# Attention, Fourier mixing and routed experts on one core: GpSimd's folds wait for VectorE, and the order of work of the sequence transform is changed

## The chip, the cores and the metric

One core of a Trainium2 chip runs the whole program in one launch. The metric is device time in microseconds; of several runs the median counts. TensorE (PE) multiplies, VectorE (DVE), ScalarE (ACT) and GpSimd (POOL) work on elements, SyncE (SP) issues most of the DMAs. Each engine works through its own list of instructions in order; semaphores (`wait_ge`, `then_inc`) tie the lists together.

## The reference

```python
scores = scale * q @ k.T; scores += slopes * -|i - j|; mask: 0 <= i - j < 128
x = softmax(scores) @ v                       # 4 x 8 heads, 576 tokens, 64 wide
...
X = fft over tokens, then over the 512 features; mixed = real(X)
u = x + mixed; un = (u - mean) / sqrt(var + 1e-6)
x = u + relu(un @ w_ch1) @ w_ch2              # 512 -> 2048 -> 512
...
e = argmax(x @ w_gate), or the last token's expert where the local gate says so
out = softmax(gate)[e] * relu(x @ w1[e]) @ w2[e]   # 8 experts, 512 -> 1024 -> 512
```

## The kernel before

Every float32 product is made of three float16 products: an operand is split into a high half, a rounded copy (names ending in `_hi`, on ScalarE), and a low half, the rest (`_lo`, on VectorE or GpSimd).

**Attention.** The 32 heads are worked on as 16 pairs (`PAIRS`), four pairs to a batch (`PPB`). Iteration p has on TensorE the scores of pair p + 1, the transposed scores of pair p, and the sums over keys of pair p - 1 (`pv`). ScalarE has the high halves of q and k of pair p + 2 (`qk_hi_of`, L1150), the exponentials (L1159, L1160), v, `x_hi_of` (L1179) and the copy of the row of maxima (`copy_row`, L1164). VectorE has `normalise(p - 2)` (L1440 to L1448), the maxima `max_of` (L1402 to L1409), `qk_lo_of(p + 2)` (L1426), `p_lo_of` (L1433) and `neg_of` (L1419, L1421). GpSimd has, in this order, `v_lo_of(p)` (L1859, after `neg_of(p)`), `x_lo_of(p - 5)` (L1867), `fold_x(p - 3)` (L1887, L1888, and a copy of an end column, L1894, for one pair in four), `fold_d(p - 4)` (L1904) and sometimes `xl_lo_of` (L1875). The folds add and subtract mirrored tokens and features of x, so that the transform needs half of the rows. SP asks, in each iteration, for v of pair p + 2 (after `v_lo_of`), four shifts of x and its store (after `normalise`), and last for q and k of pair p + 3 (L525, after `qk_lo_of(p + 2)`).

**The transform along the sequence.** For each batch b, `spectrum(b)` (L838) makes two chunks on TensorE, numbered k = 2b + c, in banks 0 and 1 or 2 and 3 of PSUM by turns; chunk k waits until `spectrum_lo` of chunk k - 2 has read its banks (`ulo_done`). `spectrum_hi` (L1226, L1229) and `spectrum_lo` (L1508, L1510) split it. `middle_rows` makes the rows of the middle feature, for batch 0 and then for the other three; `middle_hi_of` and `middle_lo_of` split them. Once batch 0 is through, `tile_spectrum(0, 4)` (L868 to L875) transforms the first tile of tokens along the features; `copy_b` and `fold` (VectorE) and `u_q` (GpSimd, L1981, after a gather of rows of x from memory, L1955) make u of it, `moments` (L1561, L1565), `std_of` (ScalarE, L1254) and `normalise_u` (L1569, L1572) normalise it, and `transpose_un` (L884) turns it for the channel MLP. `edge()` (L957, L961) makes the last sums for the rows at a batch's edge, after a small transpose of the gate's weights (L987).

**The channel MLP.** `mlp(t)` works through 9 tiles of 2 x 128 tokens (`hidden` L908, `project` L925). Its weights arrive in 32 chunks of 512 columns, staged in a ring of 10 buffers; `w_hi_of(n)` (L1218) and `w_lo_of(n)` (L1454) split chunk n, and SP's `load_w(n)` (L530) waits for the split of chunk n - 10. `mlp(0, first=True)` waits for the chunks as it comes to them: 4 ahead of `hidden(0, 0)`, 8 ahead of `hidden(0, 2)`, 10 ahead of `project(0, 0)`, 16 ahead of `hidden(0, 4)`. Behind it come the other tiles, the routing and the experts, none of which the diff touches.

The order on each engine is written out by hand; nothing plans it.

Of the kernel before, what the change touches and what calls it, by code (L numbers as in the profile page):

```python
# [32 lines left out]
B, NH, S, DH = 4, 8, 576, 64  # L33
# [7 lines left out]
PAIRS = HEADS // 2  # L41
# [76 lines left out]
def fused_kernel(nc, qk, v, mlp_w, exp_w, w_gate, bias, seq_dft, dim_dft, ident, ident_b,  # L118
# [9 lines left out]
    with ctx:  # L128
# [381 lines left out]
        def settle(engine):  # L510


            engine.sem_inc(passed, 1)
# [148 lines left out]
        def _(pe):  # L662
# [304 lines left out]
            pe.wait_ge(table_made, 3)  # L967
            pe.wait_ge(table_clear, 2)
            spectrum(0, (0,))
            for a in range(2):  # L970
                pv(PAIRS - 1, a)
            pe.wait_ge(p_lo[0], PAIRS)
            spectrum(0, (1,))
            pe.wait_ge(x_done, PAIRS)
            pe.wait_ge(xl_split, 1)
            middle_rows(1)
            spectrum(1)
            pe.wait_ge(ulo_done, DH2)
            pe.wait_ge(middle_split, 1)
            tile_spectrum(0, 4)  # L980
# [2 lines left out]
            middle_rows(B)  # L983
            spectrum(3)
            transpose_un(0, 4, un_first)
            pe.wait_ge(ulo_done, DH2 * B)
            nc.tensor.transpose(psum[0:DC * (E + 1), 0, 0:P], wg_in.rearrange("p c e -> p (c e)"), ident_sb[:, :])\  # L987
                .then_inc(gateT_ready, 1)
            pe.wait_ge(middle_split, 2)
            edge()  # L990
            mlp(0, first=True)
# [145 lines left out]
        def _(act):  # L1137
# [74 lines left out]
            def w_hi_of(n):  # L1212
                act.wait_ge(w_loaded[n % WRING], 16 * (n // WRING + 1))
                at = W_ORDER[n]
                if at >= W_FREE and n == min(W_ORDER.index(i) for i in range(W_FREE, WCH)):
                    act.wait_ge(x_split, PAIRS)
                    act.wait_ge(xl_split, B)
                nc.scalar.activation(wparts[:, 0, at * CH:(at + 1) * CH], w_staging[n % WRING], ACT.Copy, scale=WS)\  # L1218
                    .then_inc(w_hi, 1)
# [20 lines left out]
                    nc.scalar.activation(mid_last[0:rows, 0, b:b + 1], psum[0:rows, 6, QUART:TH], ACT.Copy, scale=own)\  # L1240
                        .then_inc(middle_hi, 1)

            for n in range(W_SPEC):
                w_hi_of(n)

            def copy_b(t, first=False, at=0):
                act.wait_ge(ab_ready, t + 1)
                if not first:
# [48 lines left out]
                hidden_hi(t, 7, first)  # L1297

            spectrum_hi(0, (0,))
            x_hi_of(PAIRS - 4)  # L1300
            spectrum_hi(0, (1,))
            x_hi_of(PAIRS - 3)
            middle_hi_of(1)
            spectrum_hi(1, (0,))
            xl_hi_of(B - 1)
            x_hi_of(PAIRS - 2)
            spectrum_hi(1, (1,))
            act.wait_ge(m_clear, 1)
            x_hi_of(PAIRS - 1)
            copy_b(0, first=True, at=4)  # L1310
            w_hi_of(4)
            spectrum_hi(2, (0,))
            w_hi_of(5)
            spectrum_hi(2, (1,))
            w_hi_of(6)
            std_of(0)
            spectrum_hi(3, (0,))
            middle_hi_of(2)
            spectrum_hi(3, (1,))
            w_hi_of(7)  # L1320
            unT_hi_of(0, at=4)
            w_hi_of(8)
            mlp(0, first=True)
            mlp(1, second=True)
# [59 lines left out]
        def _(dve):  # L1384
# [97 lines left out]
            for p in range(PAIRS):  # L1482
                more = p + 1 < PAIRS
                if p > 1:
                    normalise(p - 2)
                if more:
                    max_of(p + 1, 0)
                if p + 2 < PAIRS:
                    qk_lo_of(p + 2)
                if more:  # L1490
                    max_of(p + 1, 1)
                p_lo_of(p, 0)
                if more:
                    max_of(p + 1, 2)
                    neg_of(p + 1)
                p_lo_of(p, 1)
            normalise(PAIRS - 2)
            normalise(PAIRS - 1)

            def spectrum_lo(b, chunks=range(DH2)):  # L1500

# [9 lines left out]
                                            psum[:, bank:bank + 2, 0:320].rearrange("p r (q g) -> p r q g", q=2)[:, :, :, 0:QUART],  # L1511
                                            part[0], ALU.subtract).then_inc(ulo_done, 1)

            def middle_lo_of(n):

                rows = 1 if n == 1 else B
                dve.wait_ge(middle_hi, 1 if n == 1 else B)
                for b in range(1) if n == 1 else range(1, B):
                    own = 1.0 if n == 1 else ident_sb[0:rows, b:b + 1]
                    part = [middle[0:rows, h, b * HALF:(b + 1) * HALF].rearrange("p (g r) -> p r g", r=2) for h in range(2)]  # L1520
                    nc.vector.scalar_tensor_tensor(out=part[1], in0=psum[0:rows, 6:8, 0:QUART], scalar=own, in1=part[0],
                                                   op0=ALU.mult, op1=ALU.subtract)
                    last = nc.vector.scalar_tensor_tensor(out=mid_last[0:rows, 1, b:b + 1], in0=psum[0:rows, 6, QUART:TH],
                                                          scalar=own, in1=mid_last[0:rows, 0, b:b + 1], op0=ALU.mult,
                                                          op1=ALU.subtract)
                last.then_inc(middle_split, 1)

            spectrum_lo(0)
            w_lo_of(0)
            w_lo_of(1)  # L1530
            dve.wait_ge(middle_clear, 1)
            middle_lo_of(1)

            def u_of(t, q):
                return u_sb[:, bass.ds(t % 2, 1), q, :].rearrange("p o d -> p (o d)")
# [18 lines left out]
                nc.vector.tensor_tensor(u[:, FC:D], summ[:, FC - 2:0:-1], xg[:, 0, FC:D], ALU.add)\  # L1554
                    .then_inc(up_done, 1)

            def moments(t):
                for q in range(2):
                    dve.wait_ge((up_done, uq_done)[q], t + 1)
                    settle(dve)  # L1560
                    nc.vector.bn_stats(bstat[:, q, :], u_of(t, q)).then_inc(stat_done, 1)  # L1561
                for q in range(2):
                    dve.wait_ge(stat_done, 2 * t + 1 + q)
                    settle(dve)
                    nc.vector.bn_aggr(mv[:, q, :], bstat[:, q, :]).then_inc(mv_done, 1)  # L1565
# [93 lines left out]
                if not last:  # L1659
                    x2_of(t, first)  # L1660

            dve.wait_ge(table_loaded, 1)
            nc.vector.memset(eps_sb[:, :], XS * XS * LN_EPS)
            spectrum_lo(1, (0,))

            def end_fold_d(n):

# [4 lines left out]
                                        ALU.add if n % 2 == 0 else ALU.subtract).then_inc(d_done, 1)  # L1672

            end_fold_d(PAIRS - 2)
            dve.wait_ge(eo_done, PAIRS)
            for par in range(2):
                dve.wait_ge(x_stored[par], 16 * PAIRS // 2)
            nc.vector.memset(bcopy[:, 0:1], 0.0)
            nc.vector.memset(bcopy[:, FC - 1:FC], 0.0).then_inc(m_clear, 1)
            w_lo_of(2)  # L1680
            spectrum_lo(1, (1,))
            end_fold_d(PAIRS - 1)
            fold(0, first=True, at=4)
            w_lo_of(3)
            spectrum_lo(2, (0,))
            w_lo_of(4)
            spectrum_lo(2, (1,))
            moments(0)
            w_lo_of(5)
            normalise_u(0, un_first)  # L1690
            spectrum_lo(3, (0,))
            middle_lo_of(2)
            spectrum_lo(3, (1,))
            unT_lo_of(0, at=4)
            for n in range(6, 9):
                w_lo_of(n)
            dve.wait_ge(gateT_ready, 1)
# [158 lines left out]
        def _(pool):  # L1856
# [71 lines left out]
            for p in range(PAIRS):  # L1928
                if p > 0:
                    pool.wait_ge(neg_ready, p + 1)  # L1930
                    for a in range(2):
                        v_lo_of(p, a)
                if p > 4:
                    x_lo_of(p - 5)
                if p > 2:
                    fold_x(p - 3)
                if p > 3:
                    fold_d(p - 4)
                if p % PPB == 3 and p > PPB:
                    xl_lo_of(p // PPB - 1)  # L1940
                if p in (1, 2):
                    table_part(p - 1)
# [215 lines left out]
```

## Time and profile before

| | us |
|---|---|
| median of 3 runs | 897.63 |
| lowest, highest | 895.72, 898.65 |
| profiled execution, its own time | 901.19 |
| its span, first to last instruction | 899.4 |
| mean granted clock of TensorE | 0.978 |

The times in the rows below are microseconds from the start of the span. "[1.24 <-DVE m_mem L1448]" behind a row means that the engine had been idle so long and what ended the idle time. In the granted clock, 1.00 is full speed.

### The profile page before, as it was taken

How to read it: one execution, taken by the hardware profiler on the slowest of the kernel's cores; microseconds unless marked ns; L12 is line 12 of the kernel's file. 1: busy time of each engine (PE TensorE's matmuls, PEld its weight loads, DVE VectorE, ACT ScalarE, POOL GpSimd, SP SyncE). 2: the span in 40 equal slices, each digit the busy share in tenths (PEclk: the TensorE clock that was granted, in tenths of full speed). 3: DMA queues.
4: the chain of work that ended last, by engine and by line, in shares of the span. 5: the costliest groups of instructions: out<-in, count | busy, mean ns of one | idle time of the engine just before them, and what ended most of it. 6: DMA issues, size and time to landing. Idle time of an engine off the chain costs nothing.

```text
span 899.4 us, 22524 instructions
## 1 busy us (share of the span) xinstructions
PE 847.5 (94%) x8820; PEld 610.3 (68%) x8821; DVE 549.4 (61%) x1123; ACT 307.2 (34%) x461; POOL 273.4 (30%) x289
## 2 busy tenths in 40 slices
PE   8989988989999999999999999929999999999995
PEld 4767767867666676767676767517777777777773
DVE  6899986887656575747484839768995883000000
ACT  5788887553111111111111111103333333333331
POOL 2457776602010101010111100013444444334431
PEclk9999999999999999999999999959999999999998
DMA  9455552654310101010101003405774772111100
GB/s 289 131 170 149 178 146 62 197 201 133 117 47 23 47 23 47 23 47 23 47 23 47 25 24 130 129 27 165 253 236 147 228 231 80 47 45 51 49 24 1
DMA packets 60474, 91.28 MB, mean 101 GB/s; under 512 B 7304, under 2 KB 30971, under 8 KB 60421
## 3 DMA queue, kind: packets, MB, share of 16 engines
q1 hardware_dynamic: 55061, 74.80, 27.0%
q0 software_dynamic: 5360, 15.74, 5.5%
q8 instruction: 37, 0.61, 0.3%
q14 instruction: 16, 0.13, 0.0%
HBM read 73.16 MB, written 16.57 MB: 100 GB/s over the span
## 4 chain that ended last, share of the span: by engine, by line
PE 80%; DVE 9%; DMA 3%; issue 2%; ACT 2%; SPq 2%; POOL 1%; DVEq 0%; POOLq 0%; ACTq 0%
PE psum L908 21%; PE psum L925 21%; PE psum L1085 14%; PE psum L1101 14%; DMA m_mem<-in_qk 2%; PE psum L675 2%; DVE m_mem L1405 1%; DVE arena L1426 1%; DVE arena L1433 1%; PE psum L1052 1%; PE psum L884 1%; PE psum L788 1%; PE psum L875 1%; PE psum L868 1%; PE psum L1034 1%
## 5 line engine op out<-in xcount | busy, mean ns | idle before, releaser
L908 PE MATMUL psum<-m_mem,arena 128*128 (+1 forms) x1728 | 198.5, 273 | 0.0
L925 PE MATMUL psum<-arena,m_mem 128*128 128x512 f16 x864 | 195.3, 379 | 0.0
L908 PEld LDWEIGHTS psum<-m_mem,arena 128*128 128x128 f16 x1728 | 169.5, 98 | 28.3 <-issue 0.4
L925 PEld LDWEIGHTS psum<-arena,m_mem 128*128 128x128 f16 x864 | 84.5, 98 | 90.4
L1085 PEld LDWEIGHTS psum<-m_mem,arena 128*128 x2400 | 137.1, 97 | 6.9 <-issue 1.5
L1085 PE MATMUL psum<-m_mem,arena 128*128 128x128 f16 x2400 | 139.4, 218 | 1.2 <-issue 0.6
L1101 PE MATMUL psum<-arena,m_mem 128*128 x600 | 133.4, 379 | 0.0
L1268 ACT ACTIVATE m_mem<-psum 128x512 f16<-128x512 f32 x72 | 43.0, 597 | 243.2 <-PE psum L908 243.2
L1615 DVE SCALAR_TENSOR_TENSOR m_mem<-m_mem,arena 128x512 f16<-128x512 f32 x144 | 102.8, 768 | 0.0
L1101 PEld LDWEIGHTS psum<-arena,m_mem 128*128 128x128 f16 x600 | 57.7, 98 | 65.1
L1987 POOL TENSOR_TENSOR arena<-m_mem,arena 128x1024 f16<-128x1024 f32 x9 | 19.2, 2135 | 256.5 <-ACT arena L1279 211.6
L1586 DVE SCALAR_TENSOR_TENSOR m_mem<-psum,m_mem 128x512 f16<-128x512 f32 x72 | 49.4, 687 | 50.3 <-ACT m_mem L1268 49.6
L675 PE MATMUL psum<-arena 64*128 64x256 f16 (+3 forms) x960 | 55.3, 253 | 15.7 <-DVE m_mem L1405 13.4
L2026 POOL TENSOR_TENSOR m_mem<-m_mem 128x1024 f32 (+1 forms) x25 | 51.2, 2046 | 51.8 <-ACT m_mem L1353 51.7
L1350 ACT ACTIVATE m_mem<-psum 128x1024 f32 (+1 forms) x25 | 25.6, 1024 | 113.1 <-PE psum L1085 113.1
L1633 DVE SCALAR_TENSOR_TENSOR arena<-dimdft_sb,arena 128x512 f16<-128x512 f32 x74 | 59.8, 808 | 2.5
L675 PEld LDWEIGHTS psum<-arena 64*128 64x128 f16 x960 | 37.8, 95 | 26.9 <-DVE m_mem L1405 16.1
L1597 DVE SCALAR_TENSOR_TENSOR m_mem<-psum,m_mem 128x512 f32<-128x512 f32 x18 | 11.6, 686 | 57.3 <-PE psum L925 57.3
L1859 POOL TENSOR_TENSOR m_mem<-arena,m_mem 128x320 f16<-128x320 f32 x32 | 25.2, 810 | 63.9 <-DVE m_mem L1421 46.3
L1631 DVE TENSOR_SCALAR arena<-dimdft_sb 128x512 f16<-128x512 f32 x74 | 35.4, 478 | 13.4 <-PE psum L1101 13.4
L1633 DVE SCALAR_TENSOR_TENSOR arena<-wstage,arena 128x512 f16<-128x512 f32 (+1 forms) x54 | 40.7, 754 | 3.5
L1362 ACT ACTIVATE m_mem<-psum,m_mem 128x512 f32<-128x512 f32 x25 | 17.2, 689 | 71.8 <-PE psum L1101 68.2
(242 smaller groups left out, 1073.0 us busy)
## 6 DMA issues: line engine op xcount, KB each, us to landing
dimdft_sb<-in_exp_w SPq DMA_DIRECT2D x74, 256.0 KB
wstage<-in_exp_w SPq DMA_DIRECT2D x54, 256.0 KB
m_mem<-in_qk SPq DMA_DIRECT2D x16, 576.0 KB, 4.5
arena<-in_mlp_w SPq DMA_DIRECT2D x24, 256.0 KB, 4.4
arena<-in_v SPq DMA_DIRECT2D x32, 160.0 KB, 2.6
x_rows<-m_mem SPq DMA_DIRECT2D x16, 320.0 KB, 3.0
x_rows<-arena SPq DMA_DIRECT2D x9, 512.0 KB, 2.8
arena<-gate_rows SPq DMA_DIRECT2D x9, 256.0 KB, 5.2
```

The costliest lines, as they stand in the source:

```text
L675: done = nc.tensor.matmul(psum[:, banks + a, cols[0]:cols[1]], qkflat[p % 3][rows, at:at + P], qkparts[p % 3][rows, other_lo, other, o0:o0 ...
L908: last = nc.tensor.matmul(psum[:, 2 + k % 4, (f % 2) * 2 * P:(f % 2 + 1) * 2 * P], w1_sb[:, sp_, c, f * P:(f + 1) * P], unT[:, bass.ds(t % ...
L925: last = nc.tensor.matmul(psum[:, 6 + q, :], hT[:, k % 4, sp_, at:at + P], w2_sb[:, mp, f, :], start=f == 0 and sp_ == 0 and mp == 0, stop ...
L1085: last = nc.tensor.matmul(psum[:, bank + f // 4, f % 4 * P:(f % 4 + 1) * P], pointed(regs[wp * EW + c * FE + f * P], P), tokens[:, mp, c, ...
L1101: last = nc.tensor.matmul(psum[:, 7 if last_bank else 6, :], heT[:, turn, sp_, f, :], pointed(regs[mp * EW + DC * FE + f * D], D), start=f ...
L1268: nc.scalar.activation(hT[:, k % 4, 0, :], psum[:, 2 + k % 4, :], ACT.Relu).then_inc(h_hi, 1)
L1350: nc.scalar.activation(heT[:, bass.ds(k % 2, 1), 0].rearrange("p o f s -> p (o f s)"), psum[:, bank:bank + 2, :].rearrange("p b n -> p (b ...
L1586: nc.vector.scalar_tensor_tensor(out=hT[:, k % 4, 1, :], in0=psum[:, 2 + k % 4, :], scalar=0.0, in1=hT[:, k % 4, 0, :], op0=ALU.max, op1=A ...
L1615: nc.vector.scalar_tensor_tensor(out=products[j % 2], in0=x2_sb[:, q, :], scalar=1.0 / XS, in1=gate_cols[e], op0=ALU.mult, op1=ALU.mult, a ...
L1631: nc.vector.tensor_scalar(hi, staging[at], WS, None, ALU.mult).then_inc(w_hi, 1)
L1633: nc.vector.scalar_tensor_tensor(out=lo, in0=staging[at], scalar=WS, in1=hi, op0=ALU.mult, op1=ALU.subtract).then_inc(w_split, 1)
L2026: nc.gpsimd.tensor_tensor(part[1], hs, part[0], ALU.subtract).then_inc(he_lo, 1)
```

## The change

It has two parts. In the attention loop GpSimd gets a wait in front of `fold_x`: it starts when VectorE's `qk_lo_of` of the same iteration is done. And the transform's work is put into another order on PE, ACT and DVE; the `spectrum_lo`, `middle_lo_of` and `moments` calls are cut into smaller pieces for it, and ScalarE gets one extra square root of one column, early, which brings the load of that function's table forward.

```diff
 # PE
             spectrum(0, (0,))
+            pe.wait_ge(p_lo[0], PAIRS)
+            spectrum(0, (1,))
             for a in range(2):
                 pv(PAIRS - 1, a)
-            pe.wait_ge(p_lo[0], PAIRS)
-            spectrum(0, (1,))
+            spectrum(1, (0,))
             pe.wait_ge(x_done, PAIRS)
             pe.wait_ge(xl_split, 1)
             middle_rows(1)
-            spectrum(1)
+            spectrum(1, (1,))
...
             transpose_un(0, 4, un_first)
-            pe.wait_ge(ulo_done, DH2 * B)
+            pe.wait_ge(ulo_done, DH2 * B - 1)
             nc.tensor.transpose(... wg_in ...).then_inc(gateT_ready, 1)
+            pe.wait_ge(ulo_done, DH2 * B)
             pe.wait_ge(middle_split, 2)
             edge()
 # ACT
-            for n in range(W_SPEC):
-                w_hi_of(n)
...
             spectrum_hi(0, (0,))
+            w_hi_of(0)
+            w_hi_of(1)
+            spectrum_hi(0, (1,))
+            w_hi_of(2)
             x_hi_of(PAIRS - 4)
-            spectrum_hi(0, (1,))
+            act.wait_ge(x_done, PAIRS - 1)
+            nc.scalar.activation(std[:, 0:1], eps_sb[:, :], ACT.Sqrt)
+            w_hi_of(3)
             x_hi_of(PAIRS - 3)
+            spectrum_hi(1, (0,))
             middle_hi_of(1)
-            spectrum_hi(1, (0,))
+            spectrum_hi(1, (1,))
             xl_hi_of(B - 1)
+            w_hi_of(4)
             x_hi_of(PAIRS - 2)
-            spectrum_hi(1, (1,))
+            x_hi_of(PAIRS - 1)
             act.wait_ge(m_clear, 1)
-            x_hi_of(PAIRS - 1)
             copy_b(0, first=True, at=4)
-            w_hi_of(4)
             spectrum_hi(2, (0,))
             w_hi_of(5)
             spectrum_hi(2, (1,))
-            w_hi_of(6)
+            middle_hi_of(2)
             std_of(0)
             spectrum_hi(3, (0,))
-            middle_hi_of(2)
+            w_hi_of(6)
             spectrum_hi(3, (1,))
+            unT_hi_of(0, at=4)
             w_hi_of(7)
-            unT_hi_of(0, at=4)
 # DVE
+            dve.wait_ge(table_loaded, 1)
+            nc.vector.memset(eps_sb[:, :], XS * XS * LN_EPS)
             normalise(PAIRS - 2)
-            normalise(PAIRS - 1)
...
-            spectrum_lo(0)
+            spectrum_lo(0, (0,))
+            spectrum_lo(0, (1,))
+            normalise(PAIRS - 1)
+            spectrum_lo(1, (0,))
+            dve.wait_ge(middle_clear, 1)
+            middle_lo_of(1, [0])
             w_lo_of(0)
             w_lo_of(1)
...
-            spectrum_lo(1, (0,))
+            spectrum_lo(1, (1,))
...
             end_fold_d(PAIRS - 2)
-            dve.wait_ge(eo_done, PAIRS)
+            end_fold_d(PAIRS - 1)
+            w_lo_of(2)
...
-            w_lo_of(2)
-            spectrum_lo(1, (1,))
-            end_fold_d(PAIRS - 1)
             fold(0, first=True, at=4)
+            spectrum_lo(2, (0,))
             w_lo_of(3)
-            spectrum_lo(2, (0,))
-            w_lo_of(4)
             spectrum_lo(2, (1,))
-            moments(0)
-            w_lo_of(5)
+            stats(0, 0)
+            middle_lo_of(2, [1, 2])
+            moments(0, first=True)
+            spectrum_lo(3, (0,))
             normalise_u(0, un_first)
-            spectrum_lo(3, (0,))
-            middle_lo_of(2)
+            middle_lo_of(2, [3])
             spectrum_lo(3, (1,))
             unT_lo_of(0, at=4)
+            w_lo_of(4)
+            w_lo_of(5)
             for n in range(6, 9):
                 w_lo_of(n)
 # POOL, in the loop over p
                 if p > 2:
+                    pool.wait_ge(qk_lo, min(p + 3, PAIRS))
                     fold_x(p - 3)
```

## Rows read from the trace of the kernel before

**Rows 1.** The page, busy time, share of the span and instructions of each engine.

```profile
PE 847.5 (94%) x8820; PEld 610.3 (68%) x8821; DVE 549.4 (61%) x1123; ACT 307.2 (34%) x461; POOL 273.4 (30%) x289
```

**Rows 2.** Busy time by stretch: limits, length, busy us of each engine, PEclk, DMA share, GB/s.

```profile
185.70:229.80 44.10, 44.10 (x307) 30.54 (x307) 29.28 (x56) 18.26 (x35) 6.72 (x8) 0.98 0.62 196
```

**Rows 3.** Timeline of VectorE: start, us, engine, line, operation, output and inputs; undisturbed iterations.

```profile
35.18 1.35 DVE L1426 SCALAR_TENSOR_TENSOR arena<-m_mem,arena 128x1152 f16<-128x1152 f32 x1
...
96.54 1.45 DVE L1426 SCALAR_TENSOR_TENSOR arena<-m_mem,arena 128x1152 f16<-128x1152 f32 x1
98.09 1.23 DVE L1405 TENSOR_REDUCE m_mem<-psum 128x4 f32<-128x1024 f32 x1
```

**Rows 4.** Timeline of GpSimd in the same iteration and the next.

```profile
96.13 0.64 POOL L1887 TENSOR_TENSOR arena<-m_mem,arena 128x256 f32<-128x256 f32 x1
96.73 1.76 POOL L1888 TENSOR_TENSOR arena<-m_mem,arena 128x256 f32<-128x256 f32 x1
98.45 1.40 POOL L1904 TENSOR_TENSOR arena<-arena 128x640 f32<-128x640 f32 x1
101.57 1.51 POOL L1859 TENSOR_TENSOR m_mem<-arena,m_mem 128x320 f16<-128x320 f32 x2 [1.72 <-DVE m_mem L1421]
```

**Rows 5.** Timelines of GpSimd (first) and VectorE, disturbed iterations.

```profile
60.75 1.41 POOL L1904 TENSOR_TENSOR arena<-arena 128x640 f32<-128x640 f32 x1
```

```profile
60.84 2.53 DVE L1426 SCALAR_TENSOR_TENSOR arena<-m_mem,arena 128x1152 f16<-128x1152 f32 x1 [0.68 <-ACT arena L1150]
...
132.05 2.56 DVE L1426 SCALAR_TENSOR_TENSOR arena<-m_mem,arena 128x1152 f16<-128x1152 f32 x1 [0.79 <-ACT arena L1150]
```

**Rows 6.** What followed: TensorE and VectorE timelines, and the stretch 64 to 68 us.

```profile
64.56 0.42 PE L675 MATMUL psum<-arena 64*128 64x192 f16 x6 [2.14 <-DVE m_mem L1405]
```

```profile
135.81 0.42 PE L675 MATMUL psum<-arena 64*128 64x192 f16 x6 [2.29 <-DVE m_mem L1405]
```

```profile
64.00:68.00 4.00, 3.44 (x43) 2.97 (x44) 3.58 (x6) 2.88 (x6) 1.24 (x2) 0.63 0.48 153
```

```profile
68.86 0.17 DVE L1440 TENSOR_SCALAR m_mem<-psum 128x10 f32<-128x10 f32 x1 [1.05 <-ACT m_mem L1164]
...
139.74 0.17 DVE L1440 TENSOR_SCALAR m_mem<-psum 128x10 f32<-128x10 f32 x1 [0.69 <-ACT m_mem L1164]
```

**Rows 7.** Timeline of ScalarE: q and k waiting for their load, and x's high half.

```profile
59.65 1.16 ACT L1150 ACTIVATE arena<-m_mem 128x1152 f16<-128x1152 f32 x1 [1.90 <-DMA m_mem<-in_qk]
...
101.47 0.75 ACT L1179 ACTIVATE arena<-arena 128x640 f16<-128x640 f32 x1
```

**Rows 8.** Timeline of TensorE in the transform: the three holes, and matmuls of the edge.

```profile
155.47 1.82 PE L778 MATMUL psum<-m_mem,arena 128*128 128x65 f16 x54 [1.24 <-DVE m_mem L1448]
...
174.57 4.73 PE L838 MATMUL psum<-m_mem,arena 128*128 128x145 f16 x72 [1.75 <-DVE arena L1510]
```

```profile
183.06 0.29 PE L987 MATMUL psum<-ident_sb,wg_in 128*36 128x128 f32 x1 [2.48 <-DVE arena L1510]
183.28 0.83 PE L957 MATMUL psum<-dimdft_sb,arena 128*4 128x257 f16 x6
...
184.16 1.18 PE L957 MATMUL psum<-dimdft_sb,arena 128*4 128x257 f16 x6
```

**Rows 9.** Timeline of GpSimd, ScalarE and VectorE: u's second half, table load, normalised tile.

```profile
173.12 1.12 POOL L1981 TENSOR_TENSOR m_mem<-m_mem 128x257 f32<-128x257 f32 x1 [0.69 <-DMA m_mem<-x_rows,xrow_sb]
...
174.23 1.28 ACT L1254 ACT_TABLE_LOAD   x1
...
178.43 1.00 DVE L1572 TENSOR_SCALAR m_mem<-m_mem 128x512 f32<-128x512 f32 x2
```

**Rows 10.** SP's queue: the weight chunks' loads, and the time to their landing.

```profile
162.70 2.34 SPq L530 DMA_DIRECT2D arena<-in_mlp_w  x3
...
169.17 9.51 SPq L530 DMA_DIRECT2D arena<-in_mlp_w  x4
```

```profile
DMA to landing us min/median/max: 2.5/4.5/7.5
```

More of the change, by code:

```diff
@@ L1512, in spectrum_lo, with middle_lo_of @@
                                             part[0], ALU.subtract).then_inc(ulo_done, 1)
-            def middle_lo_of(n):
+            def middle_lo_of(n, of):
                 rows = 1 if n == 1 else B
                 dve.wait_ge(middle_hi, 1 if n == 1 else B)
-                for b in range(1) if n == 1 else range(1, B):
+                for b in of:
                     own = 1.0 if n == 1 else ident_sb[0:rows, b:b + 1]
@@ L1525, in middle_lo_of @@
                                                           op1=ALU.subtract)
-                last.then_inc(middle_split, 1)
-            spectrum_lo(0)
+                if of[-1] in (0, B - 1):
+                    last.then_inc(middle_split, 1)
+            spectrum_lo(0, (0,))
[4 more added lines that the diff above has]
+            middle_lo_of(1, [0])
             w_lo_of(0)
             w_lo_of(1)
-            dve.wait_ge(middle_clear, 1)
-            middle_lo_of(1)
             def u_of(t, q):
@@ L1555, in fold, with stats, moments @@
                     .then_inc(up_done, 1)
[L1557 to L1561, printed above, removed]
+            def stats(t, q):
+                dve.wait_ge((up_done, uq_done)[q], t + 1)
+                settle(dve)
+                nc.vector.bn_stats(bstat[:, q, :], u_of(t, q)).then_inc(stat_done, 1)
+            def moments(t, first=False):
+                for q in range(1 if first else 0, 2):
+                    stats(t, q)
                 for q in range(2):
@@ L1660, in mlp @@
                     x2_of(t, first)
-            dve.wait_ge(table_loaded, 1)
-            nc.vector.memset(eps_sb[:, :], XS * XS * LN_EPS)
-            spectrum_lo(1, (0,))
+            spectrum_lo(1, (1,))
             def end_fold_d(n):
```

## The prediction

> **What bounds the kernel now.** I read the page first. TensorE is busy 94% of the span [rows 1], so where it is full only fewer TensorE nanoseconds would help, and the diff changes no matmul. Busy time by stage comes next: from 185.7 us, the start of the first tile of the channel MLP, TensorE has no idle time for the whole stretch shown [rows 2]. What a change ahead of that point saves therefore arrives at the end nearly one for one, and what it does behind it is covered. That leaves the 185.7 us in front, in two stages.
>
> Stage one is attention (to about 152.8 us). It repeats once per pair of heads, 8.2 us each when undisturbed. The rows of VectorE and GpSimd, laid beside each other, show two lengths of `qk_lo_of` (L1426): 1.35 us alone and 1.45 us beside a short GpSimd add, but 2.53 to 2.56 us when GpSimd's `fold_d` (L1904, 1.40 us) began just before it [rows 3, 4, 5]. Four of the ten instances after 52.8 us are of the long kind (starts 60.84, 71.08, 113.92, 132.05; the second and third have 2.43 and 2.48 us). In the reverse order it is GpSimd that is held: its 128x256 subtract takes 1.76 us in place of 0.64. The chain of waits says where the lateness starts: ScalarE's first half of q and k waits for the load of q and k, up to 2.3 us; one such wait is in [rows 7].
>
> Stage two is the transform along the sequence (152.8 to 185.7 us). TensorE stands still three times: 1.24 us before the last sums over keys (`pv`), 1.75 us before `spectrum(3)`, 2.48 us before the gate transpose and `edge` [rows 8]. Each ends with VectorE.
>
> **The new wait of GpSimd.** In each iteration p from 3, `fold_x` and what is queued behind it on GpSimd (`fold_d`, the copy of the end column, `xl_lo_of`, then the next pair's `v_lo_of`) start only when `qk_lo_of(p + 2)` is done. First the gain. Four collisions at about 1.15 us each above 1.35 are 4.6 us. Does VectorE's next step want that time? `max_of(p + 1, 1)` needs TensorE's scores as well. In an undisturbed iteration these end at 98.07, just after `qk_lo_of`, so removing the 0.1 us of contention there is worth nothing [rows 3]. In the long ones the scores were ready first (61.5 against 63.3 us), so the 1.15 us count. There is a second term: after two of the four TensorE had idled 2.14 and 2.29 us, its granted clock then fell to 0.63 of full in one window (a mix of the 2.4 and 1.2 GHz levels), the transposed bias came late, and VectorE's `normalise` waited 1.05 and 0.69 us for the copied row of maxima [rows 6]. With max 1.15 us earlier the idle time is about 1.0 us, like ordinary gaps here that kept the clock. That adds 1.7 us, together 6.3. ScalarE takes 0.5 back: from its start at 59.65 us it needs until about 67.1 before the row is copied, half a microsecond after VectorE would ask; and the load of the following pair another 0.2 or so. I take 5.5 us for the profiled execution.
>
> The long `qk_lo_of` is the 1.35 us plus what was left of `fold_d` [rows 5]. The Trainium skill, "SBUF — State Buffer", section "Who interferes with whom", has the rule behind that: an operation of VectorE with both inputs in SBUF and a GpSimd operation that reads SBUF exclude each other for a whole instruction, whoever starts first. The rows agree, and the rule speaks against the second part of the change: VectorE's adds in `fold(0)` have both inputs in SBUF, and in the new order they fall beside `x_lo_of(14)` and (15) on GpSimd. By the rule up to 1.4 us would be lost there and the sum would come to 894.3 in place of 892.9. I leave it out of the sum, since the late landing below bounds the same step.
>
> Then the cost. GpSimd has to get through `fold_x` (about 1.24), `fold_d` (1.40) and now and then 0.2 to 0.5 more, before `neg_of` asks for the next `v_lo_of`. From the end of `qk_lo_of` at 97.9 that gives 100.6 to 101.1; the next call comes at 101.5, where GpSimd had been idle 1.72 us [rows 4]. ScalarE's `x_hi_of` needs `fold_d` too, and started at 101.47 [rows 7]: cover of 0.4 to 0.8 us. SP's shifts and `normalise` want only the fold of an iteration earlier. So I cost the push at nothing, its bounds being 0 and, without the cover, 0.5 us in each of 11 iterations.
>
> **The transform, step by step.** PE: `spectrum(0, (1,))` fills the first hole. Its input parts are long split and its bank is free once `p_lo_of(15, 0)` has read it at 152.04. `pv` then runs 156.6 to 158.3, and all up to the first tile's step ends at 165.75 in place of 166.85: 1.1 us earlier (the 1.24, less a slot on VectorE). The cover here is thin: `normalise(15)` now ends at 159.9 behind two `spectrum_lo`, used at 160.7; `middle_lo_of(1)` ends at 163.75, used at 164.2.
>
> ScalarE: the load of the square root's table (1.28 us, at 174.23 [rows 9]) moves to about 158.7, behind `x_hi_of(12)`. It hid in idle time before, and there it delays the first `spectrum_hi(1)` by 0.7 us, which nothing asks for until 165.75. Cost nothing. The weight chunks' halves (about 0.6 us each) are spread between.
>
> The late point: `w_hi_of(4)` now stands ahead of `x_hi_of(14)` and the rest. Its chunk is asked for by SP at 162.70 [rows 10], now 0.4 us later because the last `normalise` is. At the median 4.5 us to landing it starts at 167.6, at the slowest seen, 7.5, at 170.6. At the median: `copy_b(0)` 169.4, `fold(0)` over at 171.6, `spectrum_lo(2, (0,))` at 172.5, so `spectrum(3)` starts at 172.5 instead of 174.57 and ends at 177.2, 2.1 us early.
>
> Then the gain is mostly given back. Statistics of the mirrored half wait for GpSimd's gathered rows, which wait for the stored x (0.4 us later): u is complete at about 175.3, the moments at 176.9. ScalarE takes `std_of(0)` before `spectrum_hi(3, (0,))`, VectorE takes `spectrum_lo(3, (0,))` before `normalise_u`. The normalised tile is ready at 180.2 (was 179.43 [rows 9]); TensorE's transposes wait 3.0 us for it. They end at 181.3, both other conditions are then true, and `edge` starts at 181.6 to 182.6 instead of 183.06. I take 1.0 us saved. Bounds: 3 us saved, if the moments are not late; 1 us lost, if w_hi_of(4)'s chunk lands at the slow end. The slower clock of `edge` and the first hidden step behind an idle stretch stays: 1.18 us for six matmuls that took 0.83 just before [rows 8].
>
> `w_lo_of(4)` and (5) move behind the transposes, so chunks 14 to 18 are asked for from 183.8 (SP's queue was held by these splits already [rows 10]). At 4.5 us to landing they are there from 188.5, and ScalarE wants the first at about 191. Nothing; if late, TensorE has about 7 us more cover before it needs sixteen chunks.
>
> **The sum.** The profiled execution takes 901.19 us (span 899.4 and 1.8 around it): 901.19 - 5.5 - 1.0 = 894.7. It is 3.6 us above the median of the three runs, 897.63. If those 3.6 us are collisions that a median run doesn't have, that run keeps 5.5 - 3.6 = 1.9 of the first term; if they are something else, all 5.5. I take 3.7, the middle: 897.63 - 3.7 - 1.0 = 892.9, say 893.0.
>
> **Rivals.** (a) The collisions are rare outside this execution, or the load of q and k sets the pace of the loop: after any late landing the next one is late as well, and the 1.15 us of an iteration are waited out behind the load. Speaks for it: ScalarE waited for that load in 9 iterations. Against: in the four cases the load had landed before VectorE stalled. Then only the transform's 1.0 and a rest of about 0.6 remain: 896.0. (b) Attention gains, the transform doesn't, as the new order trades one late step (`spectrum_lo`) for another (`normalise_u`) and loses 0.3, between my 1.0 saved and the bound of 1 lost: 897.63 - 3.7 + 0.3 = 894.2. (c) On the other side: held GpSimd becomes the bound. If its folds end after `neg_of` instead of before, `v_lo_of`, then SP's loads behind it, then the next q and k load are all late, in every iteration. The push is about 0.75 us, the cover 1.2 to 1.7; it decides once folds plus push pass 1.2 us. At 0.5 us over in each of 11 iterations it gives 5.5, less 1.0: 902.1. Speaks for it: the load is already what ScalarE waits for, so nothing behind it absorbs the delay.
>
> **How the numbers follow.** The forecast with both gains 0.45, (a) 0.27, (b) 0.16, (c) 0.12. The measurement tells 0.3%, 2.7 us: faster is under 894.9, slower over 900.3. The forecast is nearly all faster, (b) mostly, (a) hardly, (c) slower: faster 0.55, same 0.34, slower 0.11. Range: from 889.5 (all 5.5 and 3 saved) to 898.5 (takes in (a) and (b) with their spread, leaves (c) out). For the likeliest case alone, 889.5 to 894.9.
>
> **What the profile would show.** Step one: L1426 near 1.35 us in every iteration, L1888 never 1.76, L1904 never just ahead of L1426; TensorE's idle time before the scores of the last tile about 1 us and the granted clock 1.0 there. GpSimd still idle ahead of L1859; if that idle is gone and ScalarE's waits for the load grow, (c) is right. Step two: no idle before `pv`; `spectrum(3)` starting about 2 us early relative to the last `p_lo_of`; one long idle before the transposes and none before `edge`; mlp(0) starting about 33.9 instead of 34.9 us after 150.81, the start of `p_lo_of(15, 0)`. What would make me wrong: a median execution without collisions, a slow landing of the fifth weight chunk, or attention paced by loads.

## The result, and the profile after

The changed kernel takes 893.14 us (median of 11 runs, 889.28 to 896.65); the kernel before, run beside it, 897.58 us (11 runs, 893.25 to 900.46). The ratio is 0.9948, 95% interval 0.9932 to 0.9964: 4.7 us less, 3.2 to 6.1. (Here and below a gain over the kernel before is worked out from the ratio, from which the plain difference of the medians, here 4.4, can be off by up to 1 us; differences between two changed kernels are those of their medians.) The forecast said 893.0. The total is as forecast, but it is made up otherwise: I had put 3.7 us down to GpSimd's wait and 1.0 to the new order. By itself the order measured 2.7 us (e2) and the wait nothing that these runs tell from zero (e1).

In the changed kernel `qk_lo_of` is L1431, the second maximum L1410, `copy_row` L1166 and `fold_d` L1915; PE's lines 838, 884, 908 and 925 are as before. Timeline of VectorE in the attention loop of the changed kernel (start, us, engine, line, idle time and what ended it):

```profile
60.40 1.36 DVE L1431 SCALAR_TENSOR_TENSOR arena<-m_mem,arena 128x1152 f16<-128x1152 f32 x1 [1.27 <-ACT arena L1152]
61.68 1.22 DVE L1410 TENSOR_REDUCE m_mem<-psum 128x4 f32<-128x1024 f32 x1
66.72 0.17 DVE L1445 TENSOR_SCALAR m_mem<-psum 128x10 f32<-128x10 f32 x1 [0.52 <-ACT m_mem L1166]
...
94.28 1.35 DVE L1431 SCALAR_TENSOR_TENSOR arena<-m_mem,arena 128x1152 f16<-128x1152 f32 x1
95.83 1.23 DVE L1410 TENSOR_REDUCE m_mem<-psum 128x4 f32<-128x1024 f32 x1 [0.20 <-PE psum L698]
...
129.40 1.36 DVE L1431 SCALAR_TENSOR_TENSOR arena<-m_mem,arena 128x1152 f16<-128x1152 f32 x1 [0.62 <-ACT arena L1152]
```

From 34 us on no `qk_lo_of` is long any more (1.34 to 1.36 us), where [rows 5] had 2.53 and 2.56 us. But the row at 60.40 waits 1.27 us for ScalarE where that of [rows 5] waited 0.68, and the copied row of maxima is late again (0.52 us at 66.72). The timeline of ScalarE says why:

```profile
59.21 1.16 ACT L1152 ACTIVATE arena<-m_mem 128x1152 f16<-128x1152 f32 x1 [2.74 <-DMA m_mem<-in_qk]
66.33 0.29 ACT L1166 ACTIVATE m_mem<-psum 128x128 bf16<-128x128 bf16 x1
```

From the landing of q and k at 59.21 ScalarE is busy without a gap until it has copied the row of maxima at 66.33. GpSimd's timeline shows the hold and what is left of the cover ahead of the next `v_lo_of` (L1870), 0.99 us:

```profile
95.71 0.64 POOL L1898 TENSOR_TENSOR arena<-m_mem,arena 128x256 f32<-128x256 f32 x1 [1.76 <-DVE arena L1431]
96.30 0.64 POOL L1899 TENSOR_TENSOR arena<-m_mem,arena 128x256 f32<-128x256 f32 x1
96.90 1.41 POOL L1915 TENSOR_TENSOR arena<-arena 128x640 f32<-128x640 f32 x1
99.31 1.50 POOL L1870 TENSOR_TENSOR m_mem<-arena,m_mem 128x320 f16<-128x320 f32 x2 [0.99 <-DVE m_mem L1426]
```

TensorE in the transform of the changed kernel:

```profile
147.30 4.73 PE L838 MATMUL psum<-m_mem,arena 128*128 128x145 f16 x72
151.86 1.82 PE L778 MATMUL psum<-m_mem,arena 128*128 128x65 f16 x54
...
168.65 4.73 PE L838 MATMUL psum<-m_mem,arena 128*128 128x145 f16 x72 [1.66 <-DVE arena L1516]
175.52 1.09 PE L884 MATMUL psum<-ident_sb,m_mem 128*128 128x128 f32 x8 [2.15 <-DVE m_mem L1585]
...
177.72 0.82 PE L957 MATMUL psum<-dimdft_sb,arena 128*4 128x257 f16 x6
...
178.70 8.03 PE L908 MATMUL psum<-m_mem,arena 128*128 128x256 f16 x72
```

The first hole of [rows 8] is gone: both steps of `spectrum(0)` run as 72 matmuls and the sums over keys follow at once. The second is 1.66 us (was 1.75). The third has moved ahead of the transposes (2.15 us, was 2.48 behind them), and nothing waits ahead of `edge`.

For all kernels of this study the span of the profiled execution splits into four stretches. The marks are starts: of `p_lo_of(15, 0)` on VectorE, of `mlp(0)` (first L908) and of the first `project` (first L925) on TensorE; the last column is the span less the third mark.

| kernel | start to p_lo_of(15, 0) | to mlp(0) | to first project | behind it |
|---|---|---|---|---|
| before | 150.81 | 34.90 | 8.91 | 704.8 |
| before, again (e9) | 146.65 | 37.23 | 8.55 | 704.6 |
| e1, wait alone | 146.52 | 35.41 | 7.87 | 704.6 |
| e2, order alone | 149.54 | 33.77 | 7.87 | 704.3 |
| e3 | 145.23 | 33.80 | 8.00 | 705.0 |
| e4 | 150.90 | 32.42 | 7.87 | 705.1 |
| changed | 146.32 | 32.38 | 7.87 | 704.3 |
| changed, again (e12) | 146.23 | 33.62 | 7.87 | 704.3 |
| e5 | 146.87 | 34.05 | 8.11 | 705.7 |
| e6 | 146.86 | 30.81 | 7.87 | 705.7 |
| e7 | 145.27 | 36.92 | 7.87 | 704.0 |
| e8 | 141.41 | 32.28 | 7.87 | 704.7 |
| e10 | 142.77 | 33.79 | 7.87 | 704.2 |
| e11 | 141.27 | 31.17 | 7.87 | 704.4 |

The last column moves by 1.7 us at most and follows neither edit: what is saved in front arrives at the end. Each row is one execution, and one kernel profiled twice differs a good deal: `before` by 4.2 us in the first column and 2.3 in the second, `changed` by 0.1 and 1.2. A difference of that size between two rows is no evidence by itself.

### The profile page after: what moved, and what is told of

Read it like the earlier page. It is cut to its first block, busy times and chain, and to the rows that moved or that the text cites. A ratio compares the mean times of both kernels' runs of the same rounds, so it can differ in the third digit from the quotient of the medians.

```text
span 890.9 us, 22533 instructions
## 1 busy us (share of the span) xinstructions
PE 842.1 (95%) x8820; PEld 606.3 (68%) x8821; DVE 542.6 (61%) x1123; ACT 307.3 (34%) x462; POOL 265.6 (30%) x289
## 4 chain that ended last, share of the span: by engine, by line
PE 80%; DVE 6%; DMA 4%; ACT 4%; SPq 3%; issue 2%; POOL 1%; DVEq 0%; ACTq 0%; POOLq 0%
PE psum L908 21%; PE psum L925 21%; PE psum L1087 15%; PE psum L1103 15%; DMA m_mem<-in_qk 3%; PE psum L1054 1%; PE psum L675 1%; ACT arena L1161 1%; ACT psum L1162 1%; DVE m_mem L1410 1%; PE psum L884 1%; SPq L563 1%; DVE arena L1438 1%; PE psum L875 1%; PE psum L868 1%
## 5 line engine op out<-in xcount | busy, mean ns | idle before, releaser
L908 PE MATMUL psum<-m_mem,arena 128*128 (+1 forms) x1728 | 197.5, 273 | 0.0
L925 PE MATMUL psum<-arena,m_mem 128*128 128x512 f16 x864 | 195.3, 379 | 0.0
L908 PEld LDWEIGHTS psum<-m_mem,arena 128*128 128x128 f16 x1728 | 169.0, 98 | 27.6 <-DVE m_mem L1594 0.2
L925 PEld LDWEIGHTS psum<-arena,m_mem 128*128 128x128 f16 x864 | 84.5, 98 | 90.4
L1646 DVE SCALAR_TENSOR_TENSOR arena<-dimdft_sb,arena 128x512 f16<-128x512 f32 x74 | 61.6, 833 | 2.5
L1644 DVE TENSOR_SCALAR arena<-dimdft_sb 128x512 f16<-128x512 f32 x74 | 33.6, 454 | 13.4 <-PE psum L1103 13.4
L1438 DVE TENSOR_TENSOR arena<-psum,arena 128x1024 f16<-128x1024 f32 x32 | 38.9, 1216 | 1.8 <-ACT psum L1162 1.8
```

What stands on the lines that cost most here:

```text
L908: last = nc.tensor.matmul(psum[:, 2 + k % 4, (f % 2) * 2 * P:(f % 2 + 1) * 2 * P], w1_sb[:, sp_, c, f * P:(f + 1) * P], unT[:, bass.ds(t % ...
L925: last = nc.tensor.matmul(psum[:, 6 + q, :], hT[:, k % 4, sp_, at:at + P], w2_sb[:, mp, f, :], start=f == 0 and sp_ == 0 and mp == 0, stop ...
L1438: nc.vector.tensor_tensor(ptparts[:, p % 2, u, 1], psum[:, 2 + 2 * u:4 + 2 * u, :], ptparts[:, p % 2, u, 0], ALU.subtract).then_inc(p_lo[u ...
L1644: nc.vector.tensor_scalar(hi, staging[at], WS, None, ALU.mult).then_inc(w_hi, 1)
L1646: nc.vector.scalar_tensor_tensor(out=lo, in0=staging[at], scalar=WS, in1=hi, op0=ALU.mult, op1=ALU.subtract).then_inc(w_split, 1)
```

## The experiments

Theory A is that of the prediction: long `qk_lo_of` instructions on the path, a transform that gains about 1 us. Theory B is its rival (a): the attention loop is paced by the loads of q and k. Ratios are to the kernel before, run beside each.

**e1: the wait alone.** The kernel before with

```diff
                 if p > 2:
+                    pool.wait_ge(qk_lo, min(p + 3, PAIRS))
                     fold_x(p - 3)
```

> The kernel before with only GpSimd's wait ahead of fold_x. Theory A (the long qk_lo_of instructions were on the path, and the wait ends them): about 3.7 us under the kernel before, 2 to 5. Theory B (the attention loop is paced by the loads of q and k, and the profiled execution of before merely was a bad one): 0 to 1 us under it. In either case qk_lo_of takes 1.35 us in every iteration of the profile; the two differ in whether the last p_lo_of comes earlier.

Measured: 897.62 us against 897.05, ratio 1.0000, 0.9982 to 1.0017. Theory A's 3.7 us is outside the interval (1.6 us gained to 1.5 lost); theory B's 0 to 1 is inside. `qk_lo_of` takes 1.34 to 1.36 us in the profile from 34 us on, so the wait ends the long ones and brings nothing that these runs tell from zero.

**e2: the order alone.** The changed kernel without that line.

> The changed kernel without GpSimd's wait, so only the new order of the transform. Theory A: 1.0 us under the kernel before, as forecast, and up to 2.5, since the two profiles show the stretch from the last p_lo_of(15, 0) to mlp(0) shorter by 2.5. Theory B: 3.5 to 4.5, all of the change's gain, with the first hidden step at the full clock in most executions. The gains of this run and of e1_wait_alone should add up to that of the change, 4.4 us.

Measured: 895.06 us, ratio 0.9970, 0.9954 to 0.9986: 2.7 us gained, 1.3 to 4.1, between the two theories. The 1.0 of my sum was too little. With e1's zero the parts add to 2.7 of the 4.7; the sum's gap of 2 lies within the intervals of the three.

**e3: only fold_d held.** In the changed kernel the wait stands ahead of `fold_d` instead:

```diff
                 if p > 2:
-                    pool.wait_ge(qk_lo, min(p + 3, PAIRS))
                     fold_x(p - 3)
                 if p > 3:
+                    pool.wait_ge(qk_lo, min(p + 3, PAIRS))
                     fold_d(p - 4)
```

> The changed kernel with the wait one step later, ahead of fold_d in place of fold_x. Theory A, in which the harm is fold_d's 1.40 us started just ahead of qk_lo_of: the same time as the changed kernel within 0.7 us; fold_x beside qk_lo_of costs GpSimd or VectorE up to 0.6 us where they meet. If holding fold_x as well is what counts: 1 to 2 us over the changed kernel. It also leaves GpSimd some 0.6 us more cover ahead of v_lo_of.

Measured: 893.91 us, ratio 0.9958, 0.9942 to 0.9973, the changed kernel's time within the intervals. No `qk_lo_of` takes over 1.57 us from 34 us on. Whatever the wait is worth, holding the long fold is enough for it.

**e4: GpSimd held longer.**

```diff
-                    pool.wait_ge(qk_lo, min(p + 3, PAIRS))
+                    pool.wait_ge(max_done[1], min(p + 2, PAIRS))
                     fold_x(p - 3)
```

> The changed kernel with GpSimd held 1.2 us longer, until the second maximum of the iteration. The profile of the changed kernel shows GpSimd idle 0.5 to 1.2 us ahead of the next v_lo_of. If that idle time is all the cover there is (my rival (c)), the push is 0 to 0.7 us beyond it in each of some 11 iterations and the loads of q and k leave later by as much: 2 to 5 us over the changed kernel. If SP's queue or the later use of v hides it, no change.

Measured: 899.59 us, ratio 1.0030, 1.0014 to 1.0046; 6.4 us over the changed kernel's median, a little more than expected, and by another way. GpSimd still waits a little before `v_lo_of` (0.15 to 0.32 us from 56 us on), and ScalarE's waits for the load are shorter in sum than in the changed kernel (10.0 us in 11 against 14.3 in 10). What grows is a cast of ten elements a partition in `neg_of` (L1424). Timelines of e4, VectorE first, then GpSimd:

```profile
91.40 1.42 DVE L1424 CAST m_mem<-m_mem 128x10 bf16<-128x10 f32 x1 [0.20 <-DVE m_mem L1414]
```

```profile
91.38 1.40 POOL L1915 TENSOR_TENSOR arena<-arena 128x640 f32<-128x640 f32 x1
```

And VectorE's group of that line, from 20 to 152 us, in e4 and in the changed kernel:

```profile
L1424 DVE CAST m_mem<-m_mem 128x10 bf16<-128x10 f32 x15 | 12.6, 840 | 3.0 <-DVE m_mem L1414 3.0
```

```profile
L1424 DVE CAST m_mem<-m_mem 128x10 bf16<-128x10 f32 x15 | 2.6, 175 | 3.0 <-DVE m_mem L1414 3.0
```

`fold_d` starts 0.02 us ahead of the cast and holds it for its whole length; over the loop that is 12.6 - 2.6 = 10 us on VectorE. The collision was moved from `qk_lo_of` to `neg_of`. My rival (c) had the sign and about the size (5.5 us in the loop), not the mechanism: the limit is the start of this cast, not that of `v_lo_of`.

**e5: the table loaded late.**

```diff
-            act.wait_ge(x_done, PAIRS - 1)
-            nc.scalar.activation(std[:, 0:1], eps_sb[:, :], ACT.Sqrt)
             w_hi_of(3)
```

> The changed kernel without the extra early square root, so that the load of its table (1.28 us on ScalarE) stands at std_of again. Theory A (the load hides in either place; in the changed kernel's profile ScalarE is idle for 3.6 us ahead of std_of): no difference from the changed kernel within 0.4 us. If it is the load's move that shortens the transform: 1.0 to 1.3 us over the changed kernel.

Measured: 893.26 us, ratio 0.9943, 0.9920 to 0.9965: the changed kernel's time. The early load of the table is worth nothing that these six runs can tell, and they tell some 2 us.

**e6: normalise_u first.**

```diff
             moments(0, first=True)
-            spectrum_lo(3, (0,))
-            normalise_u(0, un_first)
             middle_lo_of(2, [3])
+            normalise_u(0, un_first)
+            spectrum_lo(3, (0,))
             spectrum_lo(3, (1,))
```

> The changed kernel with VectorE's normalise_u and the last middle_lo_of ahead of both spectrum_lo of batch 3, into the 1.1 us for which VectorE is idle there. Theory A (the one hole left before the transposes is normalise_u's lateness): the transposes start 1.2 us earlier, edge 0.8 us earlier, 0.8 us under the changed kernel. If the last spectrum_lo sets edge instead: no difference or 0.3 us over.

Measured: 891.88 us, ratio 0.9936, 0.9915 to 0.9957; 1.3 us under the changed kernel's median, the intervals overlap. TensorE's timeline of e6 agrees with theory A:

```profile
174.26 1.09 PE L884 MATMUL psum<-ident_sb,m_mem 128*128 128x128 f32 x8 [0.76 <-DVE m_mem L1585]
175.19 0.27 PE L988 MATMUL psum<-ident_sb,wg_in 128*36 128x128 f32 x1
175.81 0.83 PE L957 MATMUL psum<-dimdft_sb,arena 128*4 128x257 f16 x6 [0.35 <-DVE arena L1516]
```

The hole of 2.15 us becomes 0.76 and 0.35.

**e7: the last sums first.** The changed kernel with TensorE's old order at its first step only:

```diff
-            pe.wait_ge(p_lo[0], PAIRS)
-            spectrum(0, (1,))
             for a in range(2):
                 pv(PAIRS - 1, a)
+            pe.wait_ge(p_lo[0], PAIRS)
+            spectrum(0, (1,))
             spectrum(1, (0,))
```

> The changed kernel with TensorE's last sums over keys ahead of the second spectrum step again, all else as changed. Theory A: the hole of 1.24 us comes back and the first tile's step is 1.1 to 1.3 us later, but the stretch behind it waits for the gathered rows of x and the moments, so 0.3 to 1.2 us over the changed kernel. If the moved step is what the transform's gain consists of: 2 us or more over it.

Measured: 896.57 us, ratio 0.9990, 0.9975 to 1.0005: 3.4 us over the changed kernel, with intervals that don't meet. That is the size of the alternative (2 us or more) and not theory A's 0.3 to 1.2, but the run is no clean test of the moved step. TensorE's timeline of e7:

```profile
149.94 1.82 PE L778 MATMUL psum<-m_mem,arena 128*128 128x65 f16 x54 [1.25 <-DVE m_mem L1453]
...
157.14 3.69 PE L838 MATMUL psum<-m_mem,arena 128*1 128x145 f16 x54 [0.81 <-DVE m_mem L1453]
...
170.53 6.35 PE L838 MATMUL psum<-m_mem,arena 128*128 128x145 f16 x72 [2.15 <-DVE arena L1516]
```

and TensorE's granted clock (0.72) in the stretch around its last row:

```profile
170.00:176.00 6.00, 5.47 (x61) 5.50 (x62) 4.36 (x12) 0.48 (x3) 1.41 (x2) 0.72 0.54 182
```

The hole of the kernel before comes back (1.25 us). The second one (0.81) stands in neither kernel. VectorE keeps the new order here, with both pieces of `spectrum_lo(0)` ahead of `normalise(15)`, and the second piece now has to wait for TensorE's sums as well. The last instruction of `normalise(15)` on VectorE, and behind it the second half of u on GpSimd, which needs the stored x, in the changed kernel:

```profile
154.28 0.82 DVE L1453 TENSOR_TENSOR m_mem<-psum,m_mem 128x640 f32<-128x640 f32 x1
```

```profile
169.74 0.73 POOL L1993 TENSOR_TENSOR m_mem<-m_mem 128x257 f32<-128x257 f32 x1 [2.63 <-DMA m_mem<-x_rows,xrow_sb]
```

and in e7:

```profile
156.26 0.82 DVE L1453 TENSOR_TENSOR m_mem<-psum,m_mem 128x640 f32<-128x640 f32 x1
```

```profile
173.36 0.73 POOL L1993 TENSOR_TENSOR m_mem<-m_mem 128x257 f32<-128x257 f32 x1 [4.38 <-DMA m_mem<-x_rows,xrow_sb]
```

Counted from `p_lo_of(15, 0)`, `normalise(15)` reaches that instruction at 7.96 us in the changed kernel and 10.99 in e7 (7.07 in the kernel before), u's second half starts at 23.42 and 28.09, and the moments are put together at 25.72 and 30.25. So e7 makes the stored x, and with it the moments, later than either kernel has them. Its 3.4 us are the price of a half-undone order, and what TensorE's moved step is worth by itself was not measured. On top, the hole before `spectrum(3)` grows from 1.66 to 2.15, and behind it the 72 matmuls take 6.35 us at a clock that fell, where they take 4.73 in the changed kernel.

**e8: q and k loaded first.** In the changed kernel SP's order within an iteration:

```diff
+                if p + 3 < PAIRS:
+                    sp.wait_ge(qk_lo, p + 2)
+                    load_qk(p + 3, (p + 1) % 2)
                 if p > 1:
                     shift_x(p - 2)
                     store_x(p - 2)
-                if p + 3 < PAIRS:
-                    sp.wait_ge(qk_lo, p + 2)
-                    load_qk(p + 3, (p + 1) % 2)
```

> The changed kernel with SP's load of q and k ahead of the four shifts and the store of x in each iteration, so that it is asked for about 1 to 2 us earlier. Theory B (the loop over pairs is paced by the landing of these loads, which is also why the wait alone gained nothing): ScalarE's waits for the load vanish and the last p_lo_of comes 2 to 5 us earlier; 2 to 5 us under the changed kernel. Theory A (paced by VectorE's own chain, the loads being late in few iterations): under 1 us.

Measured: 888.93 us, ratio 0.9905, 0.9884 to 0.9927; 4.2 us under the changed kernel, with intervals that don't meet. That is what theory B forecast (2 to 5). SP's queue in one iteration, first of the changed kernel, where q and k are asked for 3.3 us behind the first shift, then of e8:

```profile
85.24 0.54 SPq L569 DMA_DIRECT2D arena<-m_mem  x1
...
88.54 0.52 SPq L525 DMA_DIRECT2D m_mem<-in_qk  x1
```

```profile
82.52 0.43 SPq L525 DMA_DIRECT2D m_mem<-in_qk  x1
83.05 0.54 SPq L569 DMA_DIRECT2D arena<-m_mem  x1
```

VectorE's timeline of e8:

```profile
83.80 1.35 DVE L1431 SCALAR_TENSOR_TENSOR arena<-m_mem,arena 128x1152 f16<-128x1152 f32 x1
85.35 1.23 DVE L1410 TENSOR_REDUCE m_mem<-psum 128x4 f32<-128x1024 f32 x1 [0.20 <-PE psum L698]
...
92.00 1.35 DVE L1431 SCALAR_TENSOR_TENSOR arena<-m_mem,arena 128x1152 f16<-128x1152 f32 x1
```

8.20 us from one to the next, through the whole loop, and no wait of ScalarE for q and k from 34 us on (14.3 us in ten waits in the changed kernel, between 30 and 150 us).

**e9: the kernel before, again.**

> The kernel before, unchanged, for a second profiled execution and to see what the comparison makes of no change. No difference within 0.15%. If the first profiled execution of before was an unlucky one, this one shows fewer than four long qk_lo_of (over 2 us) and ends attention before 149.5 us; if the four are usual, again three to five and an end near 150.8.

Measured: 897.64 us against 898.02, ratio 0.9994, 0.9972 to 1.0016. Its profile has two long `qk_lo_of` (2.33 and 2.38 us), not four, and ends attention 4.2 us earlier than the first one. VectorE's timeline of e9, the first of the two:

```profile
60.10 2.33 DVE L1426 SCALAR_TENSOR_TENSOR arena<-m_mem,arena 128x1152 f16<-128x1152 f32 x1 [0.96 <-ACT arena L1150]
```

**e10: the early load without the wait.** e8 less GpSimd's wait.

> The kernel with the early load of q and k (e8_load_before_shift), without GpSimd's wait. Theory A (the wait is worth the collisions it ends, which lie on VectorE's chain once the loads don't pace): 1.5 to 4 us over e8_load_before_shift. Theory B (with punctual loads VectorE reaches qk_lo_of before fold_d starts, so there are no long collisions to end): within 1 us of e8_load_before_shift, qk_lo_of at 1.4 to 1.5 us and never at 2.5.

Measured: 890.37 us (889.21 to 890.71), ratio 0.9924, 0.9902 to 0.9946; 1.4 us over e8 by the medians, between the theories; the intervals overlap. Its profile has one long `qk_lo_of` (2.53 us at 51.42) and 1.49 to 1.50 us in all later ones, and ends attention 1.36 us later than e8.

**e11: both edits that helped,** e6 and e8 together.

> The changed kernel with both edits that helped: q and k loaded ahead of the shifts, and normalise_u ahead of the last two spectrum_lo. If they are independent (attention, transform) the gains add: 0.8 to 1.3 us under e8_load_before_shift, about 887.8 us.

Measured: 887.20 us (886.35 to 889.78), ratio 0.9897, 0.9873 to 0.9921. 1.7 us under e8's median (the intervals overlap), 9.2 us under the kernel before: the fastest of the study.

**e12: the changed kernel, again.**

> The changed kernel, unchanged, for a second profiled execution, and so that e10 to e12 stand beside it on the same chip. 4 to 5 us under the kernel before; the stretch from the last p_lo_of(15, 0) to mlp(0) again 32.4 us, within 0.5.

Measured: 893.66 us, ratio 0.9957, 0.9940 to 0.9974: as in the first comparison. The stretch to `mlp(0)` was 33.6 us, not 32.4: in this execution `edge` ran at the lower clock, and it lies outside the half microsecond that I had allowed.

## Why the prediction came out, and where its steps were wrong

**The wait: collisions ended, term too large.** It ends the long `qk_lo_of` (e1, changed kernel), and the folds cost VectorE nothing in their new place. But the 3.7 us for a median execution did not come: 0 in e1, and by the medians of the changed kernel and its repetition against e2, which were not run side by side, 1.4 to 1.9. The step that failed is "the 1.15 us count": I compared VectorE only with TensorE's scores, and gave rival (a), in which the 1.15 us "are waited out behind the load", 0.27. e8 shows that the loads pace the loop: asked for earlier, they end ScalarE's waits and bring 4.2 us. When one lands late, ScalarE starts late, works without a gap and hands over the row of maxima late, and a VectorE that is earlier waits for it, as at 66.72. In e1's profile VectorE waits for that row seven times (2.8 us in all), in the two profiles of the kernel before three times (2.0) and twice (0.7).

The other failed step is the reading of one execution. For the profiled one I forecast 5.5 us, and 150.81 to 146.32 is 4.5, but the kernel before got to 146.65 in e9 without any change, so that near hit was luck. Nor do the long instructions alone set the length: two of them went with 146.65 us in e9 and with 149.54 in e2. What the wait is worth by itself stays open between 0 and 2 us. With punctual loads it was 1.4 us by the medians and 1.36 in the profile's first stretch (e10 against e8), with intervals that overlap.

**The cover of the push.** "Cost nothing" held. Its edge is 0.5 to 1.2 us away in the idle time before L1870 (from 55 us to 135), as I read it, but the price beyond (e4) is paid by a cast in `neg_of`, which I had not looked at.

**The transform: steps right, clock left out.** Step by step against the first profile, in times from `p_lo_of(15, 0)`: the first tile's step on TensorE is over 1.3 us earlier (forecast 1.1), the chunk of `w_hi_of(4)` was taken up at 16.35 us (forecast 16.8), `spectrum(3)` starts 1.4 us earlier (forecast 2.1), the moments are ready at 26.1 us (forecast 26.1), un is ready 0.5 us later than before (forecast 0.8), `edge` starts 1.95 us earlier (forecast 0.5 to 1.5), `mlp(0)` 2.5. "Then the gain is mostly given back" is open: e7 was meant to test it and doesn't, as its edit delays the moments themselves. In the changed kernel and in e7 alike ScalarE's `std_of(0)` waits for the moments, and `spectrum_hi(3, (0,))`, `spectrum_lo(3, (0,))` and `normalise_u` stand in line behind it, as I had said.

What I priced at nothing was the clock. "The slower clock of `edge` and the first hidden step behind an idle stretch stays", I wrote. In this pair of profiles it didn't: `edge` takes 1.86 us where it took 2.43, and the stretch from `mlp(0)` to the first `project` 7.87 where it took 8.91. That is 1.6 us beside the 1.95 of `edge`'s earlier start.

Over all profiles the clock is a matter of how often. In the four with the sums ahead of the second spectrum step (before, e9, e1, e7) it fell at least once between `spectrum(3)` and the first `project`; in the ten of the new order it fell in five (e2, e3, e5, e10, e12) and stayed in five, the two with the smallest hole before the transposes (0.76 us, e6 and e11) among them. Before `spectrum(3)` the holes were 2.06 to 2.27 us in e9, e1 and e7, and its 72 matmuls took 6.31 to 6.35 us; behind 1.75 us in the first profile of before, and 1.30 to 1.69 in all ten of the new order, they took 4.73.

TensorE's stretch from `p_lo_of(15, 0)` to the first `project` is 43.3 to 45.8 us in three profiles of the old order and 40.1 to 41.8 in the seven with the new order as changed (e2, e3, e4, e8, e10 and two of the changed kernel): 3 us shorter, where e2's times give 2.7, 1.3 to 4.1. How much of this is holes closed and how much the clock was read from profiles only; no run holds one of them fixed.

**The rule left out of the sum.** VectorE's first add of `fold(0)` in the changed kernel, with GpSimd's `x_lo_of` beside it:

```profile
165.64 1.75 DVE L1563 TENSOR_TENSOR m_mem<-m_mem 128x257 f32<-128x257 f32 x1
167.32 0.41 DVE L1564 TENSOR_TENSOR m_mem<-m_mem 128x255 f32<-128x255 f32 x1
```

```profile
164.33 2.77 POOL L1878 TENSOR_TENSOR arena<-arena 128x640 f16<-128x640 f32 x2
```

Nearly the same add takes 0.41 us when GpSimd is through; this one is over soon after GpSimd's pair ends at 167.10. Being held cost VectorE 1.3 us, more than the 0.7 us by which `spectrum(3)` came later than forecast, and near the 1.4 that I had named and left out. That agrees with the Trainium skill, "SBUF — State Buffer", section "Who interferes with whom". The total doesn't show it, among larger terms of either sign.

**The table load.** Forecast at nothing, measured at nothing (e5).

So that 893.0 was met is luck: the order was put too low by 1.7 us (by e2's middle value) and the wait too high, by 1.7 if it is worth what the whole change has over e2, and by 3.7 if it is worth what e1 says. In the total the two errors cancelled. Two slips in the working changed nothing: nine `qk_lo_of` lie behind 52.8 us, not ten, and "all 5.5 and 3 saved" gives 889.1, not 889.5.

## What to carry to other kernels

When one instruction of an iteration is sometimes long, ask first what starts the iteration: here the long instruction sat on a loop paced by a load, and moving the load up in SP's queue brought more than twice what removing the long instruction did. Take one execution as a sample: a second profile of the unchanged kernel would have halved the collisions that my term counted, before any edit. Holding back one engine to keep it off another's instruction can just move the meeting, so look at what it meets next, down to casts of ten elements, and count a hole in TensorE's work with what the clock does behind it. And when one step of a new order is put back to see what it was worth, follow what the other engines' orders, left as they are, make of it: in e7 they delayed the stored x by 3 us.

## What the runs showed of the hardware that I had not expected

- A VectorE cast of 128x10 elements, 0.17 us alone, took 1.42 us with a GpSimd add of 128x640 started 0.02 us ahead of it; over 15 casts the mean was 0.84 us (e4).
- Idle stretches of TensorE of nearly equal length ended differently. Behind 2.15 to 2.16 us ahead of the transposes the clock then fell in e2, e3, e10 and e12 (`edge`'s first six matmuls took 1.46 us in e2 and e12) and did not in the changed kernel's first profile (0.83), e4 and e8. Part of the spread from run to run may lie there; that wasn't tested.
